# Listing the first two expert tiles from five token tiles, routing inside the first product, and four weight subtractions on GpSimd

## The reference, cut to what matters

```python
# 1. attention with a 16-wide window and block summaries, 8 heads -> x (2, 768, 512)
# 2. routed experts, 8 experts of 512 -> 1024 -> 512
logits = x @ w_gate;  local_gate = sigmoid(x @ w_local)
for b in range(B):
    for s in range(S):
        fresh_e = argmax(logits[b, s])
        e = fresh_e if s == 0 or local_gate[b, s] < 0.5 else prev_e
        prev_e = e
        out[b, s] = softmax(logits[b, s])[e] * (relu(x[b, s] @ w1[e]) @ w2[e])
# 3. theta = x @ w_theta; y = w_tok_r @ (x cos theta) + w_tok_i @ (x sin theta)
#    u = x + y;  out = u + relu(u @ w_ch)
```

## Time and profile before

| | |
|---|---|
| median of three runs | 424.63 us |
| profiled execution | 423.96 us |
| its span | 422.2 us |
| TensorE busy | 409.2 us, 97% of the span |
| VectorE busy | 258.0 us, 61% |
| ScalarE busy | 194.1 us, 46% |
| GpSimd busy | 80.8 us, 19% |
| granted TensorE clock | 0.999 of full speed |

### The profile page before, as it was taken

The page is one execution under the profiler, slowest core; times in us unless marked ns, Lnnn a source line. Parts: engine busy times, 40 slices in busy tenths (PEclk is TensorE's granted clock), DMA queues, the critical chain, the costliest instruction groups (busy, mean ns, idle before and its releaser), DMA issues.

```text
span 422.2 us, 8097 instructions
## 1 busy us (share of the span) xinstructions
PE 409.2 (97%) x2791; PEld 328.6 (78%) x2792; DVE 258.0 (61%) x429; ACT 194.1 (46%) x431; POOL 80.8 (19%) x127
## 2 busy tenths in 40 slices
PE   6889999999999999999999999999999999999996
PEld 3668786468888888888888778888888888888885
DVE  4898998898646327363117595666687646454352
ACT  1698995624647326463247464444433143213110
POOL 3697783221112100121110023200000000000000
PEclk9999999999999999999999999999999999999999
DMA  8995551162989933518130025300000000000012
GB/s 293 412 374 170 185 178 78 51 249 73 380 274 397 367 153 90 208 35 338 50 100 26 0 72 202 100 2 0 0 2 0 26 25 0 27 25 27 25 57 93
DMA packets 17424, 54.50 MB, mean 129 GB/s; under 512 B 2033, under 2 KB 2161, under 8 KB 17137
## 3 DMA queue, kind: packets, MB, share of 16 engines
q1 hardware_dynamic: 12560, 40.98, 27.1%
q0 software_dynamic: 2960, 9.70, 7.0%
q10 hardware_dynamic: 1872, 3.41, 2.1%
HBM read 40.46 MB, written 13.63 MB: 128 GB/s over the span
## 4 chain that ended last, share of the span: by engine, by line
PE 77%; DVE 3%; ACT 3%; DVEq 1%; issue 1%; ACTq 0%; POOL 0%
PE ps L1570 15%; PE ps L1572 14%; PE ps L1571 14%; PE ps L1714 8%; PE ps L1715 8%; PE ps L1716 8%; PE ps L1652 2%; PE ps L1592 2%; PE ps L1621 2%; PE ps L1460 2%; ACT w_h L756 1%; PE ps L1565 1%; DVE w_l L1095 1%; PE ps L1432 1%; DVEq L1102 1%
## 5 line engine op out<-in xcount | busy, mean ns | idle before, releaser
L1714 PE MATMUL ps<-z_h,mix_h 128*128 128x512 f32 x144 | 56.9, 395 | 0.0
L1716 PE MATMUL ps<-z_h,mix_l 128*128 128x512 f32 x144 | 56.1, 390 | 0.0
L1715 PE MATMUL ps<-z_l,mix_h 128*128 128x512 f32 x144 | 56.1, 390 | 0.0
L1570 PE MATMUL ps<-w_h,hT_h 128*128 128x512 f32 x104 | 42.0, 404 | 0.8 <-DVE w_l L1095 0.5
L1095 DVE TENSOR_TENSOR w_l<-w_raw,w_h (+1 forms) x32 | 37.4, 1219 | 8.3 <-ACT w_h L756 8.3
L705 ACT ACTIVATE p<-s,nmax 128x120 f32<-128x120 f32 x96 | 36.5, 384 | 11.1 <-DVE nmax L938 11.1
L1572 PE MATMUL ps<-w_l,hT_h 128*128 128x512 f32 x104 | 40.7, 391 | 0.0
L1571 PE MATMUL ps<-w_h,hT_l 128*128 128x512 f32 x104 | 40.5, 390 | 0.0
L1570 PE MATMUL ps<-w_h,xT_h 128*128 128x512 f32 x96 | 38.4, 400 | 0.0
L1571 PE MATMUL ps<-w_h,xT_l 128*128 128x512 f32 x96 | 37.4, 390 | 0.0
L1572 PE MATMUL ps<-w_l,xT_h 128*128 128x512 f32 x96 | 37.4, 390 | 0.0
(11 more groups left out here) (264 smaller groups left out, 860.2 us busy)
## 6 DMA issues: line engine op xcount, KB each, us to landing
w_raw<-w SPq DMA_DIRECT2D x32, 512.0 KB, 6.2
mix_raw<-mix SPq DMA_DIRECT2D x6, 768.0 KB, 6.0
kfull<-k_full SPq DMA_DIRECT2D x8, 400.0 KB, 6.4
q_all<-q_t SPq DMA_DIRECT2D x6, 512.0 KB, 7.3
vpad<-v_pad SPq DMA_DIRECT2D x4, 768.0 KB, 8.8
xd<-x_sb POOLq DMA_DIRECT2D x12, 256.0 KB, 4.6
ys<-y_sb ACTq DMA_DIRECT2D x12, 256.0 KB, 2.0
out<-o SPq DMA_DIRECT2D x12, 256.0 KB, 2.0
```

The costliest lines, as they stand in the source:

```text
L1570: pe.matmul(ps[:, bank, :], a_h[:, k, :], w_h[:, n, :], start=(k == 0), stop=False)
L1714: pe.matmul(ps[:, i, :], w_h, zh, start=(jb == 0 and m == 0), stop=False)
L1715: pe.matmul(ps[:, i, :], w_h, zl, start=False, stop=False)
L1716: mm = pe.matmul(ps[:, i, :], w_l, zh, start=False, stop=(jb == TPB - 1 and m == 1))
```

## The change

Six things are changed.

1. `FROM = TPB - 1 = 5`: the first two slot tiles are listed from the first five token tiles of batch 0. All `o_...` tensors shrink from six columns to five. Every step of the `first_...` chain moves a token tile earlier on VectorE and TensorE, so that `first_ranks`, `first_lanes` and `first_list` lie inside tile 11 of the attention loop, ahead of `norm(11)`. The full routing counts the tokens of expert 0 in five tiles with one more matmul.
2. GpSimd starts the gather of slot tile 0 ahead of its wait for `norm(11)`.
3. Five of the six `keep_warm` matmuls between the last logits and the first product go, and the routing visits of TensorE are moved into the first product: the turn after its first matmul, the back after its second, the ranks after its fifth.
4. `routing_list` goes from ahead of `product1(1)` to ahead of its last quarter; `transpose_slots(2)` goes from ahead of `product2(0)` to its middle.
5. VectorE subtracts quarters 0 and 1 of w1 and 2 and 3 of w2; GpSimd subtracts quarters 2 and 3 of w1 and 0 and 1 of w2, ahead of `r_ot`.
6. Copies move: both `pT` copies of tile 10 stand at the head of VectorE's tile, the second one of tile 11 goes to ScalarE, ScalarE does two quarters of `w1_h` ahead of `xaT_copy(11)`, and VectorE's `xT_copy(1)` stands in the middle of the routing.

```diff
 FIRST_TILES = 2
+FROM = TPB - 1
-WARM, WARM_SUM, WARM_SLOTS = (5, 1), (1, 0), (3, 1, 1, 1)
+WARM, WARM_SUM, WARM_SLOTS = (5, 1), (1, 0), 1
...
             for g in range(NT):
+                if g == NT - 1:
+                    pool.wait_ge(x0_saved, 16 * TPB)
+                    pool.wait_ge(olist_done, 1)
+                    load_first(0)
                 pool.wait_ge(norm_done, g + 1)
...
-            pool.wait_ge(x0_saved, 16 * TPB)
-            pool.wait_ge(olist_done, 1)
-            load_first(0)
             pool.wait_ge(xTf_ready, 1)
             load_first(1)
+
+            def rest(i, raw, hi, lo, hi_done, done):
+                pool.wait_ge(hi_done, i + 1)
+                pool.tensor_tensor(lo[:, i * SW:(i + 1) * SW, :], raw[:, i * SW:(i + 1) * SW, :],
+                                   hi[:, i * SW:(i + 1) * SW, :].bitcast(f32), ALU.subtract).then_inc(done, 1)
+
+            pool.wait_ge(w1_split, STEPS + STEPS // 2)
+            for i in range(STEPS // 2, STEPS):
+                rest(i, w1_raw, w1_h, w1_l, w1_hi, w1_split)
+            for i in range(STEPS // 2):
+                rest(i, w2_raw, w2_h, w2_l, w2_hi, w2_split)
             pool.wait_ge(tiles_ready, 1)
...
-                if 1 < g <= SUMMARY_TILES:
+                if 1 < g <= SUMMARY_TILES or g == NT - 1:
                     pT_copy(g, 1)
...
-            xaT_copy(NT - 1)
-            act.sem_inc(xTf_h, 1)
             act.wait_ge(scores_ready, NT)
             for i in range(STEPS):
+                if i == STEPS // 2:
+                    xaT_copy(NT - 1)
+                    act.sem_inc(xTf_h, 1)
...
+                if g == NT - 2:
+                    pT_copy(g, 0)
+                    pT_copy(g, 1)
+                if g == NT - 1:
+                    first_ranks()
+                    first_lanes()
                 inverse(g, s)
-                if g == NT - 2:
-                    first_keys()
...
-                if g == NT - 2:
+                if g == NT - 3:
                     first_scan()
-                if g == TPB + 2:
+                if g == FROM + 2:
                     first_logits(g - 2)
...
-                if g == NT - 3:
+                if g == FROM + 3:
                     first_other()
+                if g == NT - 2:
+                    first_choice()
                 if g == NT - 1:
-                    first_choice()
+                    first_list()
                 norm(g)
...
             lg_copy(NT - 2)
-            first_ranks()
-            first_lanes()
+            w1_step(0)
             lg_copy(NT - 1)
-            first_list()
...
-            w1_step(0)
+            w1_step(1)
             dve.wait_ge(vT_ready, 1)
...
-            w1_step(1)
             dve.wait_ge(count_ready, 1)
...
+            xT_copy(1)
             rank = ps[:, B_R, R_RANK:R_RANK + E * NT].rearrange("p (e j) -> p e j", e=E)
...
-            w1_step(2)
-            xT_copy(1)
             dve.wait_ge(list_ready, 1)
...
-            w1_step(3)
             hT_copy(0)
-            for i in range(STEPS):
+            dve.wait_ge(w2_split, STEPS + STEPS // 2)
+            for i in range(STEPS // 2, STEPS):
                 split_step(i, i, w2_raw, w2_h, w2_l, w2_hi, w2_split)
...
+                if g == NT - 1:
+                    first_rank()
                 transpose_p(g, s, first)
+                if g == NT - 2:
+                    first_back()
...
-                if g == NT - 2:
+                if g == NT - 3:
                     first_turn()
                 if g == NT - 1:
-                    first_back()
+                    first_list()
                 weigh(g, first)
...
-            keep_warm(WARM_SLOTS[0])
-            routing_turn()
-            keep_warm(WARM_SLOTS[1])
-            routing_back()
-            keep_warm(WARM_SLOTS[2])
             transpose_slots(0, first=True)
-            keep_warm(WARM_SLOTS[3])
-            routing_ranks()
+            keep_warm(WARM_SLOTS)
...
                     mm = pe.matmul(ps[:, B_H + c, :], xT_f[:, k, :], w1_raw[:, k * SW + c, :], start=(k == 0), stop=(k == KD - 1))
-                    if c == 1 and k == 1:
+                    if (c, k) == (0, 0):
+                        routing_turn()
+                    if (c, k) == (0, 1):
+                        routing_back()
+                    if (c, k) == (1, 0):
+                        routing_ranks()
+                    if (c, k) == (1, 1):
                         transpose_slots(1)
...
-            routing_list()
-            product1(1, 0)
-            transpose_slots(2)
-            product2(0, 0, first=True)
+            product1(1, 0, middle=routing_list)
+            product2(0, 0, first=True, middle=lambda: transpose_slots(2), at=KF // 2)
```

More of the change, by code:

```diff
@@ L156, in program @@
         overlay = at[0]
[L157 to L174, removed]
+        o_lg = sb("o_lg", [P, FROM, E + 1])
+        o_m = sb("o_m", [P, FROM])
+        o_t = sb("o_t", [P, FROM])
+        o_u = sb("o_u", [P, FROM])
+        o_f = sb("o_f", [P, FROM])
+        o_v = sb("o_v", [P, FROM])
+        o_scan = sb("o_scan", [FROM, P])
+        o_carry = sb("o_carry", [P, FROM + 1])
+        o_w = sb("o_w", [P, FROM], i32)
+        o_e = sb("o_e", [P, FROM], i32)
+        o_oe = sb("o_oe", [P, FROM], bf16)
+        o_cum = sb("o_cum", [P, FROM], bf16)
+        o_off = sb("o_off", [P, FROM])
+        o_slot = sb("o_slot", [P, FROM], u32)
+        o_tile = sb("o_tile", [P, FROM], u32)
+        o_lane = sb("o_lane", [P, FROM], u32)
+        o_in = sb("o_in", [P, FROM, FIRST_TILES])
+        o_ot = sb("o_ot", [P, FROM, FIRST_TILES], fp16)
         at[0] = overlay
@@ L1062, in first_list, with split_step, w1_step @@
                 dve.tensor_copy(slot_list[:, 0:FIRST_TILES], ps[:, B_O, P + 24:P + 24 + FIRST_TILES]).then_inc(olist_done, 1)
+            def split_step(n, i, raw, hi, lo, hi_done, done):
+                dve.wait_ge(hi_done, n + 1)
+                dve.tensor_tensor(lo[:, bass.ds(i * SW, SW), :], raw[:, bass.ds(i * SW, SW), :],
+                                  hi[:, bass.ds(i * SW, SW), :].bitcast(f32), ALU.subtract).then_inc(done, 1)
+            def w1_step(i):
+                split_step(i, i, w1_raw, w1_h, w1_l, w1_hi, w1_split)
             dve.memset(warm, 1.0).then_inc(warm_done, 1)
@@ L1120, in hT_copy @@
                                       hT_h[:, c * 4:c * 4 + 4, :].bitcast(f32), ALU.subtract).then_inc(hT_taken, 1)
-            def w1_step(i):
-                split_step(i, i, w1_raw, w1_h, w1_l, w1_hi, w1_split)
             count = [0]
@@ L1572, in product, with product1 @@
                 return pe.matmul(ps[:, bank, :], a_h[:, k, :], w_l[:, n, :], start=False, stop=(k == last))
-            def product1(t, place):
+            def product1(t, place, middle=None):
                 pe.wait_ge(xTf_taken, t + 1)
@@ L1577, in product1 @@
                 for k in range(KD):
+                    if middle and k == KD - 1:
+                        middle()
                     pe.wait_ge(w1_split, place * STEPS + (STEPS + k + 1))
@@ L1593, in transpose_h, with product2 @@
                 mm.then_inc(hT_ready, 1)
-            def product2(t, place, first=False, middle=None, bank=B_Y):
+            def product2(t, place, first=False, middle=None, at=KF // 4, bank=B_Y):
                 if not first and bank == B_Y:
@@ L1598, in product2 @@
                 for k in range(KF):
-                    if middle and k == KF // 4:
+                    if middle and k == at:
                         middle()
```

68 lines of the change are left out of this document (31 added, 37 removed).

## The result

The changed kernel takes **429.11 us**, the median of ten runs (427.26 to 432.05). The kernel before, on the same chip, took 424.38 us, also the median of ten (424.07 to 425.94). The ratio is 1.0114, 95% interval 1.0093 to 1.0135, so it is 4.7 us slower. The prediction was 423.9 us with a range of 422.0 to 426.2. The profiled execution took 429.68 us, its span is 427.9 us, and its mean granted clock is 0.991.

A forecast was written before the change was run, and what follows sets the result against it. From 101.7 us TensorE bounds the kernel. `product1(2)` was to start at 101.74 less 4.85, plus 0.6, 0.95, 0.3, 0.55, 0.55 and 1.1, so 101.0: 0.7 us gained, 423.9 us, range 422.0 to 426.2.

The forecast's parts named there:

- the wait for the ranks: In the first product, after five matmuls: PE waits from 80.35 us until `r_cum` ends at 81.3, +0.95 us.
- First product: Earlier list and gather let the first product start at about 75.55 us, 4.85 us earlier.
- The duration: Each of GpSimd's four 1024-element subtractions takes 1.9 us: 1.7 plus 0.2 of fixed cost.
- rival A: GpSimd's subtractions are longer, in series with the table chain, and the change is slower: 425.0 to 427.5 us; chance 0.22.
- `product1(1)`, list, slots, table: Later PE waits: +0.3 us at `product1(1)`, +0.55 at the list, +0.55 at slot tile 2's transposes, +1.1 at the table.
- Slack at the table: `table` ends at 100.62 us, 1.1 us ahead of the matmuls waiting for it: all the second chain's slack.
- Attention, taken as 0: Moved copies and small first-list operations in the attention loop cost 0 us, bounds -0.3 and +0.5.
- The stretch behind does not change: From 101.7 us to the end, nothing of the change reaches the stretch except when it starts.
- Rival B: The subtractions hardly block VectorE's chain, stalls nearly go and only the table wait is left: -2.5 us, 422.1; chance 0.26.
- C: GpSimd starts its subtractions late, at 79.5 to 80.3 us instead of 76.85: +0.6 to +1.2 us, 425.5; chance 0.1.
- D: The first gather doesn't move as said, half the 4.85 us is kept, time near the one before, 424.7; chance 0.08.

The follow-up runs named there:

- Run 6: Changed kernel with one-input GpSimd copies of the same size in place of the four subtractions, the rest `w_l` of these quarters left out; 425.17 us.
- run 2: Kernel before with GpSimd's four subtractions added behind its second gather, nothing else; 434.48 us.
- Run 3: Changed kernel with four `keep_warm` matmuls ahead of the ranks and two ahead of the wait for the table; 427.9 us.
- run 1: Changed kernel with all four GpSimd subtractions given back to VectorE; 428.85 us.
- run 4: Changed kernel with only one quarter (w1's third) left on GpSimd, the other three back on VectorE; 425.73 us.
- run 7: Run 4 with the ranks one matmul earlier in the first product and two `keep_warm` matmuls in the wait for the table; 426.01 us.
- run 11: Run 7 with one `keep_warm` less, all quarters on VectorE, list a quarter earlier, `xT_copy(1)` behind `r_lane`, `xT_copy(2)` behind the table; 422.64 us.
- run 5: Changed kernel with `product1(2)` taking constant place 0, ahead of the wait for the table; 429.33 us.
- run 14: Run 11 with TensorE's ranks of the first list behind the transposes of tile 11; 422.9 us.
- Run 9: Run 2 with GpSimd's subtractions started only behind VectorE's `r_al`; 431.7 us, one run.
- run 8: Kernel before with only the list from five token tiles, the earlier first gather and the moved copies, every quarter on VectorE; 425.55 us.
- run 12: Kernel before with `xT_copy(2)` behind the table, nothing else; 424.72 us.
- run 13: Run 11 with GpSimd's four subtractions put back in, nothing else; 428.42 us.

## Why the prediction was wrong

The predicted `product1(2)` was 0.7 us early; it is 4.1 us late. The step that failed is the wait for the ranks, "+0.95": it was 3.40 us, and it brought the lower clock with it. Step by step, times in the profiled execution:

- **First product, right.** Forecast 75.55, measured 75.65; the gather started at 70.50 (forecast 70.65). But this was counted as a gain of 4.85 us to be eaten up piece by piece, when VectorE's chain had not moved at all: `r_carry` at 78.12 and 78.13, where the forecast had it at 77.75.
- **The duration, mis-sized.** 1.9 us was taken for a subtraction and 2.34 measured (four in 9.33 us). By the prediction's own rule, 0.4 us for each 0.1, that is 1.8 us. This is past the deciding point of rival A, 2.1 us, but would have given only some 425.7 us, inside the range. Run 6, with pieces of 1.0 us and the same order, shows the same lever from the other side. The estimate from the Trainium skill ("GPSIMD Engine Reference", "Performance versus the Vector engine"), 2.25 us, was within 4% of it, and the 0.42 us that `r_ol` lost was too small a measure: 252 elements at the measured rate are 0.58 us. The 0.2 us of fixed cost that the sum added to it has no row.
- **The ranks: this step failed by a whole subtraction.** I let `r_e` through for nothing, `r_oe` behind the first and `r_cum` behind the second subtraction. `r_e` itself waited for the first boundary (0.77 us), so `r_oe` waited for the second and `r_cum` for the third. PE waited 3.40 us and not 0.95, and went on at 84.27 instead of 81.3. Of these 3.0 us, 2.05 are the step from the forecast's second boundary to its third (81.05 to 83.1), and 0.8 come from the longer pieces (the third boundary was at 83.9). The section "Who interferes with whom" ("SBUF — State Buffer") of the Trainium skill, from which I had taken only the case of two SBUF inputs, names `tensor_scalar` too: it can enter a 2-port mode, in which it contends with GpSimd, and the one issued later is blocked fully. The trace agrees on the effect: 0.77 us here and 9.83 in run 2. It does not show the mode.
- **The clock, not counted.** The 3.40 us without a matmul were followed by 3 us at 0.50, +1.57 us on four matmuls. The forecast had no such wait in it, so it had no reason to look; with the larger one the reason was there. Run 3 gives 1.8 us ahead of `product1(2)` and 1.3 behind.
- **`product1(1)`, list, slots, table.** Forecast 86.1, 91.2, 95.9, 100.95; measured 90.45, 95.1, 99.57, 104.75. The delay of the ranks and the clock passes down, with nothing new: VectorE waited for the list (2.63 us) and for `xT_h` (1.91) and was not the bound there.
- **Slack at the table: there was none.** I read 1.1 us from `table` to `product1(2)` as slack. The distance is 1.12 us before, 1.13 after, 1.10 or 1.11 in runs 1, 3, 4, 6, 7 and 11. In run 5, where the place is a constant, `product1(2)` starts 1.12 us ahead of the table's end without a wait. So it is the way from the table to the first matmul that reads its place from it. The forecast's 100.95 should have given 102.05, and with that alone the sum was +0.3 us, no change.
- **Attention, taken as 0:** +0.62 us, above the bound of 0.5. Some 0.44 us of it lie in tile 11, where PE waits 0.45 us for the ranks of the first list; run 14 moved this wait and did not win the time back, so the chain as a whole is in the way there. 0.3 us lie between `norm(7)` and `norm(8)` where small operations of the first choice now stand, and tile 10 gives 0.16 back.
- **"The stretch behind does not change": wrong** by 1.56 us, the clock behind the wait for the table.

The stages add up: −0.7 forecast, +4.75 for the stage, +0.6 attention, +1.6 rest, −0.5 from the start make the +5.7 us of the two spans. The +4.9 us between the forecast's `product1(2)`, 101.0, and the measured one, 105.88, are +3.0 at the ranks, +1.6 of clock behind them and +1.1 from the table to the matmul, less 0.7 us of forecast waits that shrank. Rival A had the sign and its mechanism (long subtractions in series with the chain), with 0.22; its size left out the extra subtraction, the clock and the table's 1.1 us. Rival B was wrong: operations that read PSUM did run free, but the three of the ranks did not. C and D did not occur: the subtractions started at 76.93 and the first gather at 70.50.

What stays open: why `r_al` in run 2 was not let in at three boundaries, when `r_e`, `r_oe` and `r_cum` got in at the next one each time. It was issued during GpSimd's gather and they during a subtraction. Run 9 has the same gather, which ends at 82.29, but its first subtraction waits for `r_al`, and there `r_al` ends with the gather after 0.42 us. So the gather alone holds it only to its own end; whether the start under a gather decides what the subtractions then do was not tried.

## What to carry to other kernels

Before work is moved to GpSimd, list VectorE's instructions that will run beside it, `tensor_scalar` ones from SBUF to SBUF included, and let each wait for the next boundary: a chain of dependent 0.2 us operations pays up to one GpSimd instruction each. By this the length of one piece counts, though no run here had the same total in shorter pieces. Count one VectorE operation more than looks needed: the first small one can be held too. A distance between a flag and the work behind it that is the same in every kernel is a latency and not slack. And an earlier start of one chain is worth nothing until the other chain's order is changed with it: here neither run 8 nor run 12 gained anything, and run 11, with both and more, gained 2.0 us.

## What the runs showed of the hardware

- GpSimd's two-input 128x1024 f32 operation took 2.34 us, the one-input copy of the same size 1.0, VectorE's 1.2.
- An int32 `tensor_scalar` of 128x16 on VectorE was held for 9.83 us through four back-to-back GpSimd instructions. Issued during a gather of GpSimd with nothing behind it, the same operation ended with the gather, after 0.42 us (kernel before, runs 8, 9 and 12).
- VectorE operations with one input in PSUM ran beside GpSimd without delay (`r_over` in run 9, 0.20 us inside a subtraction, as in the kernel before).
- A wait of PE of 3.40 or 4.21 us was followed by TensorE's lower clock level for 3 us or more in both cases. One of 2 us was in some executions only: in run 4 the wait was 1.97 us and the mean clock 0.999, but five of its ten runs had 0.995 or 0.996 and took 425.96 to 427.01 us, the other five 424.77 to 425.5. That the wait was the same in the runs without a trace is assumed.
- From the last table operation to the first matmul whose place is read from the table: 1.09 to 1.13 us in 13 of the 15 profiled kernels that read it there. In the other two (runs 12 and 13, 1.75 and 2.94) PE's own order came later.
